# A third pair of query copies, ScalarE's sums and first weight halves gathered ahead of the third burst, and the first batch's last keys earlier

## What is computed

```python
scores = scale * np.matmul(z, z.transpose(0, 2, 1))     # z: 8 x 3072 x 64, scale 1/3072
attn = np.maximum(scores, 0.0) ** 2
out = np.matmul(attn, v)                                # v: 8 x 3072 x 256
x = u * out                                             # then, as 24576 rows of 256:
logits = x @ w_gate                                     # 256 x 8
expert_idx = np.argmax(logits, axis=1)
for i in range(N):                                      # first come, first served
    e = expert_idx[i]
    if counts[e] < capacity:
        disp[e, counts[e]] = x[i]; pos[i] = counts[e]; counts[e] += 1; keep[i] = True
h = np.maximum(np.einsum('ecd,edf->ecf', disp, w1), 0.0)   # N here is 3072: the capacity is 768
y = np.einsum('ecf,efd->ecd', h, w2)
out[i] = gate_w[i] * y[expert_idx[i], pos[i]]           # rows that were not kept stay 0
```

## Time and profile before

| | |
|---|---|
| median of three runs | 862.79 us (861.81 to 864.39) |
| the profiled execution | 863.23 us, its span 861.4 us |
| TensorE busy | 834.5 us, 97% |
| VectorE busy | 630.0 us, 73% |
| ScalarE busy | 567.0 us, 66% |
| GpSimd busy | 170.4 us, 20% |
| DMA | 107.90 MB, mean 125 GB/s |

### The profile page before, as it was taken

The page is one execution under the profiler, slowest core; times in us unless marked ns, Lnnn a source line. Parts: engine busy times, 40 slices in busy tenths (PEclk is TensorE's granted clock), DMA queues, the critical chain, the costliest instruction groups (busy, mean ns, idle before and its releaser), DMA issues.

```text
span 861.4 us, 25760 instructions
## 1 busy us (share of the span) xinstructions
PE 834.5 (97%) x8414; PEld 667.3 (77%) x8414; DVE 630.0 (73%) x1354; ACT 567.0 (66%) x866; POOL 170.4 (20%) x204
## 2 busy tenths in 40 slices
PE   6899999999999979999999999999999999999997
PEld 5778778788888868778788888887777777777776
DVE  7886877889989858887888888777554655565521
ACT  7877776778877758776878787678534434435422
POOL 3002112112221203202302311210121221211212
PEclk9999999999999989999999999999999999999999
DMA  7923244264334733233324425722616325415101
GB/s 290 377 80 113 55 156 179 59 187 166 118 86 128 264 88 110 84 99 110 120 78 131 139 60 156 284 61 73 156 44 167 115 68 159 143 46 152 55 18 37
DMA packets 109399, 107.90 MB, mean 125 GB/s; under 512 B 68749, under 2 KB 95578, under 8 KB 108352
## 3 DMA queue, kind: packets, MB, share of 16 engines
q1 hardware_dynamic: 100640, 87.29, 33.0%
q0 software_dynamic: 8736, 20.31, 6.7%
HBM read 40.03 MB, written 44.93 MB: 99 GB/s over the span
## 4 chain that ended last, share of the span: by engine, by line
PE 72%; issue 6%; DVE 6%; ACT 6%; DMA 5%; SPq 3%; DVEq 1%; ACTq 1%; POOL 0%; POOLq 0%
PE Sc L893 15%; PE O L760 11%; PE Sc L725 11%; PE O L764 10%; PE O L762 10%; PE O L916 3%; PE O L918 3%; PE O L920 3%; DMA xT<-xrow 2%; SPq L303 2%; DVE attn_hi L1052 2%; PE Sc L918 2%; PE Sc L916 2%; PE Sc L920 2%; ACT attn L533 2%
## 5 line engine op out<-in xcount | busy, mean ns | idle before, releaser
L760 PE MATMUL O<-vS,attn_hi 128*128 128x256 f16 x1332 | 363.4, 273 | 1.7 <-DVE vS L1036 1.7
L762 PE MATMUL O<-vS,attn_hi 128*128 128x256 f16 x1332 | 363.1, 273 | 0.0
L764 PE MATMUL O<-vS,attn_lo 128*128 128x256 f16 x1332 | 363.0, 273 | 0.0
L533 ACT ACTIVATE attn<-Sc 128x768 f32<-128x768 f32 x226 | 179.6, 795 | 61.5 <-PE Sc L725 58.3
L1058 DVE TENSOR_TENSOR attn_lo<-attn,attn_hi 128x768 f16<-128x768 f32 x224 | 214.4, 957 | 6.5
L537 ACT ACTIVATE attn<-attn 128x768 f32<-128x768 f32 x225 | 189.5, 842 | 10.1 <-ACT xT L508 2.9
L1052 DVE CAST attn_hi<-attn 128x768 f16<-128x768 f32 x224 | 125.0, 558 | 58.2 <-ACT attn L537 48.1
L760 PEld LDWEIGHTS O<-vS,attn_hi 128*128 128x128 f16 x1332 | 130.1, 98 | 29.3 <-issue 11.7
L764 PEld LDWEIGHTS O<-vS,attn_lo 128*128 128x128 f16 x1332 | 130.3, 98 | 15.2
L762 PEld LDWEIGHTS O<-vS,attn_hi 128*128 128x128 f16 x1332 | 130.3, 98 | 14.2
L1368 DVE SCALAR_TENSOR_TENSOR rawv<-Sc,rawv 128x768 f16<-128x768 f32 x63 | 60.2, 956 | 110.5 <-ACT rawv L646 61.2
(11 more groups left out here) (167 smaller groups left out, 1025.0 us busy)
## 6 DMA issues: line engine op xcount, KB each, us to landing
out<-empty SPq DMA_DIRECT2D x16, 1536.0 KB, 5.9
wraw<-in_moe_w SPq DMA_DIRECT2D x16, 1024.0 KB
rawv<-in_v SPq DMA_DIRECT2D x14, 768.0 KB, 7.9
ubuf<-in_u SPq DMA_DIRECT2D x19, 384.0 KB, 3.2
disp<-vS SPq DMA_DIRECT2D x8, 774.0 KB, 11.5
rawz<-in_z SPq DMA_DIRECT2D x3, 768.0 KB
q_now<-zP POOLq DMA_DIRECT2D x18, 96.0 KB, 4.2
q_now<-zQ POOLq DMA_DIRECT2D x18, 96.0 KB, 4.2
```

Of the source, the lines that this page charges most:

```text
L533: act.activation(attn_place(c), score_place(c), ACT.Relu).then_inc(s["relu_done"], 1)
L760: nc.tensor.matmul(o_part(t), hi, v[:, 0:D], start=c == 0 and j == 0 and t % 2 == 0, stop=False, skip_group_check=True)
L762: nc.tensor.matmul(o_part(t), hi, v[:, D:2 * D], start=False, stop=False, skip_group_check=True)
L764: ins = nc.tensor.matmul(o_part(t), lo, v[:, 0:D], start=False, stop=c == PAIRS - 1 and j == 1, skip_group_check=True)
```

## The change

It does five things.

1. A third pair of copies, `q_last`, serves pair 11, so that `q_now` serves pairs 3 to 10 and is read last in the second burst. GpSimd refills `q_now` right behind that burst, ahead of its wait for the scattered rows; `q_last` and `q_next` are refilled behind the third burst. TensorE waits for `loaded_q_last` at c = 8. That makes two more DMAs of 96 KB in each group and two more ahead of the loop.
2. ScalarE's four sums of a group stand together at c = 7, behind the square of pair 10 and ahead of the Relu of pair 11. The four high halves of weights stand there too, all in group 8. Branches at c = 8, 9 and 10 go.
3. VectorE's maxima over the second expert's weights stand at c = 8 in groups 8 to 11.
4. In group 0, ScalarE makes one half of the last keys at c = 0 ahead of the Relu of pair 3, and the other at c = 1 ahead of the square of pair 4. VectorE makes its low half ahead of the piece of v.
5. In group 0 the gate's maximum and weights are made at c = 5 and 7.

```diff
+        q_last = [sb(f"q_last{k}", [P, GROUP], F16) for k in range(2)]
...
             queries(q_now, 1, "loaded_q_now")
+            queries(q_last, 1, "loaded_q_last")
             queries(q_next, 2, "loaded_q_next")
...
                 def rest():
+                    wait_apart(pool, s["scores_ready"], n * PAIRS + PAIRS - 1)
+                    queries(q_now, n + 1, "loaded_q_now")
                     wait_apart(pool, s["scattered"], n * 48)
                     pool.sem_inc(s["row_free"], 1)
...
                     wait_apart(pool, s["scores_ready"], n * PAIRS + PAIRS + BURST - 1)
-                    queries(q_now, n + 1, "loaded_q_now")
+                    queries(q_last, n + 1, "loaded_q_last")
                     queries(q_next, n + 2, "loaded_q_next")
...
                             v_hi(UNIT * (2 + V0_AT.index(c)), UNIT * (2 + V0_AT.index(c)))
+                        if peeled and c in LAST_KEYS_AT:
+                            z_hi(3 * SLICE * P, 1, c == LAST_KEYS_AT[1], SLICE * P)
...
-                        if peeled and c == LAST_KEYS_AT:
-                            z_hi(3 * SLICE * P, 1, False, SLICE * P)
-                            z_hi(3 * SLICE * P, 1, True, SLICE * P)
...
-                    if c in SUM_AT:
+                    if c == SUMS_AT:
                         def sums():
-                            q = (g & 2) * 2 + SUM_AT.index(c)
                             wait_apart(act, s["loaded_zv"], (n & 120) * 10 + 80)
                             act.wait_ge(s["logits_ready"], n)
-                            v_sum(q, q * UNIT, UNIT).then_inc(s["vsum_done"], 1)
-                            wait_apart(act, s["vsum_done"], (n & 120) + (g & 2) * 2 + SUM_AT.index(c) + 1)
+                            for q in range(UNITS // 2):
+                                at = (g & 2) * 2 + q
+                                v_sum(at, at * UNIT, UNIT).then_inc(s["vsum_done"], 1)
+                                wait_apart(act, s["vsum_done"], (n & 120) + at + 1)
...
                         if c < PAIRS:
-                            ins = scores(n, c, par)
+                            ins = scores(n, c, par, q_last if c == PAIRS - 1 else q_now)
                         else:
-                            ins = scores(n + 1, c - PAIRS, 0 if peeled else None)
+                            ins = scores(n + 1, c - PAIRS, 0 if peeled else None, q_next)
...
                             if not peeled:
+                                wait_apart(pe, s["loaded_q_last"], n * 32)
                                 wait_apart(pe, s["loaded_q_next"], n * 32)
...
-SUM_AT = (6, 7, 8, 9)
+SUMS_AT = 7
...
-W_MAX1_IN = ((8, 8), (9, 9), (10, 9), (11, 6))
-W_HI_IN = ((8, 7), (8, 8), (8, 10), (9, 10))
+W_MAX1_IN = ((8, 8), (9, 8), (10, 8), (11, 8))
+W_HI_IN = ((8, 7), (8, 7), (8, 7), (8, 7))
...
-FIRST_ACT = (6, 7, 8, 9, 10)
+FIRST_ACT = (6, 7)
...
-GATE_AT = (8, 10)
+GATE_AT = (5, 7)
...
-LAST_KEYS_AT = 1
+LAST_KEYS_AT = (0, 1)
```

More of the change, by code:

```diff
@@ L223, in relu2_attention_moe @@
             y_scattered3 fac_ready h_first hh_first due_ready loaded_early
-            loaded_q_now loaded_q_next loaded_k_next weighed counts_read"""
+            loaded_q_now loaded_q_last loaded_q_next loaded_k_next weighed counts_read"""
         s = {n: sem(n) for n in names.split()}
@@ L700, in wait_keys, with scores @@
                         pe.wait_ge(s[key], value * 8)
-            def scores(n, c, par):
+            def scores(n, c, par, copied):
                 def key_cols(z16, k_first, r):
@@ L707, in key_cols, with query_cols @@
                     return k_first[half(r), c * P:(c + 1) * P] if par is None else z16[half(r), par * S + at:par * S + at + P]
-                def query_cols(z16, q_first, q_rest, r):
+                def query_cols(z16, q, r):
                     if isinstance(n, int):
                         return z16[half(r), n * GROUP:(n + 1) * GROUP]
-                    return (q_first if par is None else q_rest)[half(r), :]
+                    return q[half(r), :]
                 high_keys, low_keys = (
@@ L716, in scores @@
                 high_queries, low_queries = (
-                    [query_cols((zP, zQ)[x], q_next[x], q_now[x], r) for x, r in ((h, 0), (1 - h, 1))] for h in range(2))
+                    [query_cols((zP, zQ)[x], copied[x], r) for x, r in ((h, 0), (1 - h, 1))] for h in range(2))
                 terms = ((high_keys, high_queries), (high_keys, low_queries), (low_keys, high_queries))
@@ L741, in _ @@
             for c in range(BURST - 1):
-                ins = scores(0, c, 0)
+                ins = scores(0, c, 0, q_next)
             ins.then_inc(s["scores_ready"], BURST - 1)
@@ L1202, in part @@
                                 ins.then_inc(s["rows_lo"], 1)
-                        if peeled and c in V0_AT:
-                            first_v(2 + V0_AT.index(c))
                         if not peeled and (c == ZLO_AT or c in VLO_AT):
@@ L1219, in part @@
                                         only_if(dve, n == 4 + q, lambda: w_max(0, 0, q))
-                        if peeled and c == LAST_KEYS_AT:
+                        if peeled and c == LAST_KEYS_AT[1]:
                             dve.wait_ge(s["zhi_ready"], 8)
@@ L1224, in part @@
                             z_lo_across(3 * SLICE * P, 1)
+                        if peeled and c in V0_AT:
+                            first_v(2 + V0_AT.index(c))
                         if not peeled and c == ROUTE_AT:
```

## The result

The changed kernel took 853.37 us (median of 4 runs, 853.07 to 854.34) beside 863.44 us for the kernel before on the same chip (4 runs, 861.81 to 864.39): a ratio of 0.9887, with a 95% interval of 0.9869 to 0.9906. That is 10.1 us less by the medians. The forecast was 850.5 us, 12.32 us less, so about a fifth of the expected gain did not come. 853.37 lies above the range of 848.6 to 852.7 us that the forecast gave to its own case, and inside the wider one, up to 854.6, that takes in its rivals. The profiled execution took 853.4 us, with a span of 851.6 us (863.23 and 861.4 before).

What follows compares the result with a forecast made beforehand. TensorE, busy 97%, was taken as the bound, so only its waits could be won. 6.66 + 4.56 + 0 + 0.93 + 0.17 = 12.32 us gave 850.5 us against the median; its own range was 848.6 to 852.7 us.

Steps and rivals of the forecast that it cites:

- Queries: Group 9's first burst: the earlier refill of q_now removes the wait and the slow clock behind it, 6.66 us.
- The rival in which `row_free` is late: GpSimd's two early copies delay gate_x in 17 groups by 0.9 us each: 866 us and over, chance 0.03.
- The clock: Group 9's slow burst, 304 to 312 us: the skill's rule gives 3.4 us back; the sum used the measured 2.1.
- Sums: Behind groups 1, 2, 9, 10 and 17: sums gathered at c = 7 remove the waits for xT, 4.56 us.
- some 1.7 us, in which a late Relu costs nothing: Sum groups: VectorE is free near 8.1 us after the third burst, while gate_x may start at 9.87.
- part 3: Group 8's weight halves gathered ahead of the Relu, and VectorE's maxima at c = 8: no cost, 0.3 and 0.5 us bounds.
- part 2: ScalarE's sums of v gathered at c = 7, to gain 4.56 us behind groups 1, 2, 9, 10 and 17.
- The forecast's own sign: TensorE's waits for xT of 0.5 us in all the sum groups would prove the blocks too long.
- the blocks outlast the pause: ScalarE, sum groups: at 2.0 us per added sum the Relu is 2.26 us late; 4 us return, 854.5 us, chance 0.12.
- Weights: Group 8: three more halves make the Relu 1.39 us late, costing nothing, bound 0.3; group 11's maxima nothing, bound 0.5.
- Keys: Group 0, Relu of pair 6: one half of the last keys fits ahead; 0.93 us goes and 1.4 stays.
- Gate: Behind group 0: earlier gate weights gain 0.17 us; the last transpose's 4.11 us stays, bound 1.5 us more gain.

Runs made afterwards that it cites:

- one branch: The changed kernel with group 8's four halves of weights under one condition ahead of the sums, in place of four branches behind them: 851.04 us.
- all three cures: The changed kernel with the weights' halves under one condition, sums written to two places in turn, scales and factor at c = 8, last maxima in group 10: 848.19 us.
- The gate's weights alone: The kernel before with only the gate's maximum and weights moved to c = 5 and 7: 863.62 us, ratio 0.9995.
- 78 turn-over matmuls: The kernel before with 78 turn-over matmuls in place of 90 ahead of the first values: 863.6 us, ratio 1.0002.
- the queries alone: The kernel before with only the third pair of query copies added: 855.73 us, ratio 0.9917.
- the sums where they were: The changed kernel with ScalarE's sums of v back at c = 6, 7, 8 and 9: 853.89 us, ratio 0.9892.
- the sums and weights alone: The kernel before with only the sums at c = 7 and the halves of the first weights in that pause: 862.92 us, ratio 0.9998.
- the keys alone: The kernel before with only the earlier last keys of group 0, at c = 0 and 1: 861.5 us, ratio 0.9981.
- the scales sooner: The changed kernel with the weights' halves under one condition, VectorE's scales and factors at c = 8, group 11's last maximum at c = 6: 849.16 us.
- 112 matmuls: The kernel with all three cures, with 112 turn-over matmuls in place of 90 ahead of the first values: 849.95 us, ratio 0.985.
- the kernel without the third pair: The changed kernel with q_now serving pairs 3 to 11 and refilled behind the third burst: 860.66 us, ratio 0.9967.

## Why the prediction was right, and where not

**Queries: right.** Priced at 6.66 us, measured 6.66 in the profile and 7.3 to 7.4 by medians. That the size fits so well is in part luck, as the other traces with the late copy lose 5.4 to 6.8 us. The copies left at 288.82 and 289.38, right behind the third scatter, with none of the register work that the forecast put between. Counted from group 8's second burst that is 9.1 and 9.7 us, where the forecast had 10.5 to 11.5. GpSimd's timeline in group 8:

```profile
287.86 0.98 POOL L448 DMA_INDIRECT disp<-xrow,slot  x1 [0.30 <-issue]
288.82 0.60 POOL L419 DMA_DIRECT2D q_now<-zP  x1
289.38 0.60 POOL L419 DMA_DIRECT2D q_now<-zQ  x1
```
```profile
q_now<-zQ POOLq DMA_DIRECT2D x1, 96.0 KB, 5.2
```

The early copy did meet traffic in this group, 5.2 us to landing where the median of all groups is 1.9; it landed at 294.56, 5.3 us ahead of the burst at 299.90. The rival in which `row_free` is late had nothing to go on: in the loop the issues of `q_now` take 0.57 to 0.76 us each, in the kernel before 0.57 to 1.20. For it the Trainium skill, in SBUF — State Buffer, section Who interferes with whom, has GpSimd shut out while VectorE holds the port that they share; these issues did not get longer. They could not have told much either, as the forecast read its row wrongly: beside the 0.58 us issue at 298.70 VectorE was not in its pause, but casting:

```profile
298.58 0.56 DVE L1052 CAST attn_hi<-attn 128x768 f16<-128x768 f32 x1 [0.91 <-ACT attn L537]
```

**The clock.** 12.37 - 10.34 = 2.0 us came back in the stretch behind the slow burst, as the burst rows had it. The Trainium skill's rule of half the throttled time, in TensorE: Matmul & The Clock Gate, section Terms, had 3.4 us here, and the trace speaks against it: TensorE stood idle for most of the first of the two stretches.

**Sums: the step that failed.** The forecast had "Two more at 1.27 are 2.54, so the Relu would be 0.80 us late" and "some 1.7 us, in which a late Relu costs nothing". It was 1.89 us late. The sums' own pace was priced right, 1.22 for 1.27, and already held one wait for the predecessor each. What was missing is the 1.01 us behind the last sum, of which the four branches are 0.73 and the last sum's own wait 0.28; without the branches the Relu would be 1.2 late. The prediction counted the halves only in group 8, where they run, and not their conditions in the groups where they don't, which stood at c = 7, 8 and 10 before. So most of the loss comes from part 3's edit and falls in part 2's groups.

The free time was less than 1.7 as well. In group 2 a Relu 1.89 late loses 0.70 us (11.04 - 10.34); with one branch it is 1.42 late and loses 0.23 (10.57 - 10.34). Both say that 1.2 us are free. The forecast had VectorE free 8.1 us after the burst if no sum is in the way. With all three cures and a Relu only 0.13 late it stands idle 0.65 us ahead of `gate_x`, which then starts at 9.49, so it is free near 8.8. And 9.49 is the earliest in any of those groups, since there `gate_x` waits for TensorE's last products.

The forecast's own sign, waits for `xT` of 0.5 us in all the sum groups, came: 0.79, 0.55, 0.53, 0.55 and 0.44. The rival "the blocks outlast the pause" had the price, 0.75 us a group for 0.73 measured (3.65 in five), and half of the mechanism. It put 2.0 us on each added sum; they take 1.22, and the register work lies in one piece behind the last. The time did not come to its 854.5, since group 1 gave 1.5 us. That gift is why 853.37 lies no further out; without it the time would have been near 854.9, above the wider range as well.

**Weights: right in group 8.** The Relu starts at 293.03 there, 3.24 behind its burst, so 0.95 late, which is free, as said. Group 11's maxima cost nothing either, in the changed kernel.

**Keys: right**, 0.81 for 0.93. **Gate: right in the term, wrong in what was left alone.** The gate's weights alone give nothing. "I see no cause in the change for it to get shorter": the transposes' 4.11 us were taken as a property of the place, and were a collision with one packet of instructions, which the change moved by accident. It was in the bounds, as 1.5 us of further gain, but that it came is luck.

So 12.32 expected, 3.7 lost on the sums, 1.5 found in group 1, 0.2 behind the scales, 0.36 more at the start, and small differences in the keys and the gate: 9.8 in the traces.

## What to carry to other kernels

Before gathering work into a pause, count everything that the sequencer must pass between the last gathered instruction and the one that is waited for, in the instances where the work is not done too: a condition not taken was 0.15 to 0.18 us here, and it is not hidden behind an instruction if a wait stands ahead of it. Where several operations in a row share a scratch target, two targets were worth more here than the new place: 1.22 us apart became 0.83, and all of the forecast gain came. And a transfer that is slow in one place only should be looked at for what shares its queues in that microsecond, before it is taken as given.

## What the runs showed of the hardware

A load of instructions, by its place TensorE's own, is 16 KB and 0.9 to 1.6 us on one transfer engine. In the five cases where it falls among three transposes the stretch is 0.4 to 1.5 us longer; 12 turn-over matmuls fewer or 22 more, somewhere else altogether, decide that.

The clock also fell at the start of some executions. With 78 turn-over matmuls TensorE stood idle longer before its first values. The stretches of that kernel:

```profile
16.00:20.00 4.00, 1.25 (x23) 1.10 (x21) 3.51 (x9) 3.94 (x6) 3.99 (x7) 1.00 0.96 365
20.00:24.00 4.00, 4.00 (x30) 2.69 (x32) 3.90 (x7) 2.90 (x4) 1.63 (x3) 0.57 1.02 410
...
32.00:36.00 4.00, 1.87 (x24) 1.48 (x26) 3.80 (x6) 3.98 (x6) 0.00 (x0) 0.73 1.03 366
36.00:40.00 4.00, 4.00 (x35) 2.88 (x32) 3.77 (x6) 2.51 (x4) 0.00 (x0) 0.84 0.94 316
```

These are means over 4 us, of time at 1.2 GHz and time at 2.4, behind one idle time near 18 us (2.75 us) and one for group 0's Relu. Against the kernel before two stretches between bursts grew by 2.02 and 1.52 us, which in this execution hid the 1.54 won in group 1. Four other traces have it too: the queries alone (0.67 and 0.70), the sums where they were (0.57 over 20 to 24 us), the gate alone (0.58 over 32 to 36) and the sums and weights alone (0.60). Their idle times near 18 us were 2.18, 1.99, 2.02 and 2.25 us. The clock stayed at 1.00 there in the kernel before, with 1.72, in the changed kernel, with 2.08, and in the keys alone, with 2.32. So whether it falls is not decided by the length of that idle time alone; what else decides it stays open.

The later fall, between 32 and 40 us, is in four of the five traces in which both halves of the last keys delay group 0's second burst, and in none of the nine with part 4 of the change. So part 4 may also spare the clock, which would explain why the keys alone gain 1.8 us by the medians for 0.8 in the trace; no run tests it. The spread of the runs may come from the same: 5.4 us over twelve runs with 78 matmuls, 5.0 over twelve with the sums and weights alone, 1.3 over four of the changed kernel, 0.5 and 0.6 over five with the scales sooner and with 112 matmuls. Only one execution of each was traced. That of the kernel without the third pair, with a clean start, took 858.6 us, 2.1 below the median of its kernel. A term of 1 us is then better read from the stretches of two traces, once the clock has been looked at, than from two medians.
